# Rounding tile sizes to 32 instead of 64 bytes in the address counter of an attention and MoE kernel

## The reference

```python
# 1: attention, two parts added
q_d, k_d, v_d = means over 4 neighbouring tokens         # 144 tokens
out_up = repeat(softmax(scale * q_d @ k_d.T) @ v_d, 4)    # pooled attention
mask = abs(pos[:, None] - pos[None, :]) < 4               # 7 neighbours
out_local = softmax(where(mask, scale * q @ k.T, -1e9)) @ v
x = (out_up + out_local) as [2304 tokens, 512]
# 2: gated product, 512 -> 1536 -> 512
y = ((x @ w_a) * (x @ w_b)) @ w_out
# 3: 512 -> 1024, softmax times its input, layer norm, -> 512
h = y @ w_in
solu = h * softmax(h)
out = (solu - mean) / sqrt(var + 1e-6) * g_ln @ w_out2
```

## Time and profile before

| | |
|---|---|
| median of three runs | 787.55 us |
| the profiled execution | 787.55 us |
| its span, first to last instruction | 785.5 us |
| TensorE busy (matmul) | 754.0 us, 96% |
| VectorE busy | 559.4 us, 71% |
| ScalarE busy | 298.3 us, 38% |
| GpSimd busy | 211.7 us, 27% |
| moved by DMA | 117.27 MB |
| mean granted clock of TensorE | 0.983 of full |

### The profile page before, as it was taken

One profiled execution on the slowest core, in us unless ns is written; L12 is line 12 of the kernel. 1 busy time (PEld: TensorE's weight loads), 2 busy tenths in 40 slices (PEclk: granted clock), 3 DMA queues, 4 the chain that ended last, 5 costly groups with the idle time before them and its releaser, 6 DMA issues.

```text
span 785.5 us, 12269 instructions
## 1 busy us (share of the span) xinstructions
PE 754.0 (96%) x4440; PEld 695.0 (88%) x4440; DVE 559.4 (71%) x975; ACT 298.3 (38%) x819; POOL 211.7 (27%) x260
## 2 busy tenths in 40 slices
PE   6778999898999999999999999999999999999998
PEld 5667889798999999999999999999988888888886
DVE  4579999979968887778687876122467766666663
ACT  3534647254353525344434424234322212222222
POOL 2458897446513421051001111122100000000000
PEclk9959999999999999999999999999999999999999
DMA  9999966595787586683955433636121011011011
GB/s 190 195 226 217 233 160 221 174 310 172 245 236 232 174 243 189 183 213 98 253 168 186 142 120 111 197 112 215 54 67 53 29 55 52 29 55 51 30 41 41
DMA packets 96652, 117.27 MB, mean 149 GB/s; under 512 B 19921, under 2 KB 59603, under 8 KB 96593
## 3 DMA queue, kind: packets, MB, share of 16 engines
q1 hardware_dynamic: 81872, 106.98, 49.2%
q10 hardware_dynamic: 14721, 9.51, 4.2%
HBM read 95.62 MB, written 20.84 MB: 148 GB/s over the span
## 4 chain that ended last, share of the span: by engine, by line
PE 84%; DVE 4%; DMA 4%; POOL 2%; SPq 2%; issue 2%; ACT 1%; ACTq 0%; DVEq 0%; POOLq 0%
PE psum L851 26%; PE psum L853 26%; PE psum L852 25%; PE psum L963 2%; DMA raw<-in_q 2%; PE psum L807 1%; POOL raw L1689 1%; PE psum L787 1%; DMA vd_scratch<-raw 1%; SPq L431 1%; PE psum L818 1%; DVE tmp L1414 1%; POOL raw L1693 1%; DMA raw<-in_v 1%; DVE tmp L1464 1%
## 5 line engine op out<-in xcount | busy, mean ns | idle before, releaser
L851 PE MATMUL psum<-x_hi,w_hi 128*128 128x384 f32 x576 | 199.0, 345 | 2.3 <-POOL w_lo L1701 2.3
L853 PE MATMUL psum<-x_hi,w_lo 128*128 128x384 f32 x576 | 194.1, 337 | 0.0
L852 PE MATMUL psum<-x_lo,w_hi 128*128 128x384 f32 x576 | 193.9, 337 | 0.0
L851 PEld LDWEIGHTS psum<-x_hi,w_hi 128*128 128x128 f32 x576 | 109.2, 190 | 5.3 <-POOL w_lo L1701 2.6
L852 PEld LDWEIGHTS psum<-x_lo,w_hi 128*128 128x128 f32 x576 | 109.3, 190 | 0.0
L853 PEld LDWEIGHTS psum<-x_hi,w_lo 128*128 128x128 f32 x576 | 109.0, 189 | 0.0
L851 PE MATMUL psum<-ab_hi,wo_hi 128*128 128x384 f32 x288 | 100.3, 348 | 3.9 <-issue 3.9
L1381 DVE TENSOR_TENSOR ab_f<-psum,a_sb 128x384 f32<-128x384 f32 x72 | 39.8, 553 | 88.1 <-PE psum L853 62.2
L853 PE MATMUL psum<-ab_hi,wo_lo 128*128 128x384 f32 x288 | 97.3, 338 | 0.0
L852 PE MATMUL psum<-ab_lo,wo_hi 128*128 128x384 f32 x288 | 97.0, 337 | 0.0
L1689 POOL TENSOR_TENSOR raw<-raw 96x256 f32<-96x256 f32 x60 | 57.3, 981 | 119.7 <-DMA raw<-in_q 53.1
(11 more groups left out here) (147 smaller groups left out, 1416.0 us busy)
## 6 DMA issues: line engine op xcount, KB each, us to landing
wo_hi<-wo_hi_scratch SPq DMA_DIRECT2D x53, 256.0 KB, 2.8
wo_lo<-wo_lo_scratch SPq DMA_DIRECT2D x53, 256.0 KB, 3.1
k_u<-in_k SPq DMA_DIRECT2D x11, 576.0 KB
v_u<-in_v SPq DMA_DIRECT2D x11, 576.0 KB
k_u<-in_k SPq DMA_DIRECT2D x17, 288.0 KB
v_u<-in_v SPq DMA_DIRECT2D x17, 288.0 KB
wo_raw<-in_moe_w_out SPq DMA_DIRECT2D x19, 256.0 KB, 4.4
raw<-in_v SPq DMA_DIRECT2D x8, 576.0 KB, 7.6
```

What stands on the lines that cost most here:

```text
L851: mm(dst, wh, xh, start=first, stop=False, skip_group_check=not check)
L852: mm(dst, wh, xl, start=False, stop=False, skip_group_check=not check)
L853: last = mm(dst, wl, xh, start=False, stop=end, skip_group_check=not check)
```

## The change

The counter of `place` rounds each tile's size up to a multiple of 32 bytes, where it rounded to a multiple of 64.

```diff
@@ -160,7 +160,7 @@
             size *= n
         if offset is None:
             offset = at["next"]
-            at["next"] = offset + (size + 63) // 64 * 64
+            at["next"] = offset + (size + 31) // 32 * 32
         return nc.alloc_sbuf_tensor_at(name, shape, dtype, offset=offset)
```

## The result

The changed kernel takes 792.0 us in the median of 12 runs (790.6 to 793.7), the kernel before 787.5 us in 12 runs beside them. The ratio is 1.0052 with a 95% interval of 1.0041 to 1.0063, 3.2 to 5.0 us. The prediction was 787.5 us and "same", with a range up to 790.4: wrong.

The account below looks back on a forecast made before the run. TensorE, busy 754.0 of 785.5 us, was taken to bound the kernel, with transfers in the head and VectorE from 50 to 150 us. 785.5 + 0 + 2.05 = 787.55 us; 8-in-10 range 785.6 to 790.4.

Parts of the forecast that it names:

- the places of the tiles: Everything behind edge moves down by 352 bytes; q_u and the tiles after it start 32 past a multiple of 64.
- bounds of the time by stage: Transfers in the head, VectorE from 50 to 150 us, TensorE's matmuls from 200 us to the end.
- Engines: Step pricing a start 32 past a multiple of 64 on the engines: 0 us, by the nearest rows.
- the upper bound: Last stage: 432 matmuls streaming win_hi or win_lo take one 64-byte unit more, 12 ns each, 5.3 us on a full TensorE.
- rival (c): Whole kernel: engines pay as well as transfers; 797.2 us; chance 0.03.
- 1.1 us on VectorE: Upper bound for operations on tmp, 60 to 150 us: 3072-byte rows take 49 units for 48, +2.1%.
- 3.2 us of transfers: Upper bound at one 64-byte unit more per run: 1.4 us in the head and 1.8 us at xup.
- Rival (a): out_d stores: 512-byte runs touch 3 blocks of 256 bytes for 2, up to 2.6 us more each; 792.7 us; chance 0.06.
- Rival (b): Head and xup: transfers pay per 64 bytes, engines do not; +3.2 us, 790.8 us at most; chance 0.05.
- Rival (d): Products of q, k, v: VectorE-GpSimd collisions fall otherwise; 2.3 us either way, 785.3 to 789.9 us; chance 0.08 over 2.4 us.
- The rule of the Trainium skill: Reads starting off a multiple of 256 bytes pay for bytes ahead; -1.2 us in the head, 0 to +3.2 at xup.

Follow-up runs that it names:

- e14: The kernel before with 384 of 512 columns in 11 of 12 w_in matmuls, and win_hi and win_lo 64 bytes higher: 768.1 us, one run.
- e15: The kernel before with 384 of 512 columns in 11 of 12 w_in matmuls, and win_hi and win_lo 32 bytes higher: 767.8 us, one run.
- e3: The kernel before with the x and y tiles 32 bytes higher and everything behind them, win among it, 64 bytes higher: 794.3 us, ratio 1.0071.
- e1: The changed kernel with win_hi and win_lo 32 bytes higher, back on a multiple of 64: 792.2 us, ratio 1.0040 to the kernel before.
- e9: The changed kernel with win_hi and win_lo 96 bytes higher, at 128 past a multiple of 256: 788.5 us, ratio 1.0002 to the kernel before.
- e8: The kernel before with win_hi and win_lo 256 bytes higher: 789.7 us, one run.
- e12: The kernel before with y_lo, and y_raw under it, alone 32 bytes higher: 791.2 us, one run.
- e10: The kernel before with win and the x and y tiles 64 bytes higher, the tiles behind x by 256: 787.5 us, one run.
- e16: The kernel before with win_hi and win_lo 64 bytes higher and full 512 columns: 790.3 us, one run.
- e2: The kernel before with only win_hi and win_lo moved, 32 bytes higher: 791.8 us, ratio 1.0042.
- e6: The kernel before with the edits of e2 and e3 together, win at 224 and y at 160 past a multiple of 256: 791.6 us, ratio 1.0052.
- e5: The kernel before, unchanged, profiled again: 786.4 us, one run.

## Why the prediction was wrong, step by step

What it said of the places of the tiles holds. Its bounds of the time by stage hold, the last stage is a full TensorE, and 7 ns there count at once.

The step that failed is the one under **Engines**: "pT_head ... is the moving operand of 32 matmuls of 96 columns: median 368 ns", against 367 ns, hence 0 for TensorE. These are plain float32 operands and 96 columns, the product with w_in is of the type FP32R and streams 512. The row was near in its place but not in its form, and the form counts: 384 columns of that type show no price in e14 and e15, and 2 ns a matmul in e3. No run separates the type from the length. What stands in the place of the 0 is 6.9 ns from start to start on each of 432 matmuls of a full TensorE, 3.0 us, and it hangs on where win lies against y within 256 bytes. No row of before on FP32R operands could show the price, because win, y, x, ab, the weight tiles and lnT all lie at 128 past a multiple of 256. That was the sign to read: where all operands of the dear product share one place, and the change takes one of them away, the trace has nothing on it, and the upper bound should weigh more.

The bound itself was sound in size: "389 / 32 = 12 ns, times 432 = 5.3 us"; measured were 7 to 8 ns and 3.1 us. It stood in rival (c), at 0.03, and beside other terms that measured nothing: 1.1 us on VectorE, 3.2 us of transfers. Its reason was wrong: no fetch of 64 bytes more, since e1 pays on a multiple of 64. That the size came near is luck.

Rival (a), the stores of out_d by blocks of 256: they landed in 5.4 us for 5.1, and e9, where out_d lies as in the changed kernel, is not slower. Its 792.7 us came near the 792.0 by luck. Rival (b), transfers by 64 bytes: refuted by e9 to within 1.3 us. Rival (d): starts of the last stage between 564.4 and 567.8 us show such shifts, but the medians agree in e9. The rule of the Trainium skill on the start of a descriptor within 256 bytes ("DMA: Bandwidth & Descriptors", "How a descriptor splits into AXI transactions") gave, as an estimate, 31% or 1.6 us on each store of out_d, so 6.7 us for 5.1. The three profiles with out_d at 160 (after, e1, e9) have medians of 5.4, 5.0 and 5.8 us, those with it at 0 between 4.5 and 5.9: the landing times do not show it. Whether more bytes are fetched, no run here shows.

Left over: 3.1 us of the product against 4.5 us between the medians. The interval reaches down to 3.2 us, and e9 leaves at most 1.3 us for all the rest.

Open is how the place of one operand lengthens the matmuls. Shown is: that a step of 256 bytes is free for this product (e8), that the weights' place counts as the streamed one's does (e12, and e3, e10 and e16 side by side), that equal places are free at 128 (e9) and nearly free at 192 (e10), and that what counts is above all the distance (e2 and e3, e6 and e16). Each of these readings rests on one profile; the times of e1, e2, e9 and of the change itself rest on 12 runs each. That the two reads collide in the memory is argued from e12, not shown, and the 395 ns of 851 there speak against its simplest form. A run without the load of weights beside the stream was not made.

## What to carry to other kernels

Give the streamed operand and the weights of a long product (here 512 columns, FP32R) the same place within 256 bytes, and pin it in the code instead of leaving it to what small tiles ahead of it take up. When a change moves addresses, list first the products on the full engine and compare their operands' places before and after; a row with another type or length says little on them. And where a mend does not bring the time back, look whether the line was mended, before another cause is taken up. Work out the addresses of all tiles after an edit of a counter, and not only of those that it was meant to move: e3 and e6 were planned on places that they did not have.

## What was not expected of the hardware

The product with w_in repeats almost exactly: from the first to the last start of L851 197.7 us in before, 197.6 in e5 and e8 and 197.7 in e9, while other places give 198.3 to 201 us, each with its own pattern over the three lines (395, 400, 389 ns in e12; 394, 388, 392 in e16; 392, 394, 388 in e6, with the same distance and the same sum as e16). A start 32 bytes past a multiple of 64 has cost the other engines and the transfers nothing that was measured (e9, to within 1.3 us).
